# A per-head state in half the columns, y in two PSUM banks, and 14 routing operations on VectorE instead of 17, in a fused attention and mixture-of-experts kernel

## The reference

```python
# 1. linear attention, B=4, H=8, S=768, D=48
cur = einsum('bhd,bhe->bhde', u * k_t, v_t)
y_t = einsum('bhd,bhde->bhe', r_t, state + cur)
state = w * state + einsum('bhd,bhe->bhde', k_t, v_t)
# 2. x = y as (3072, 384); 8 experts, the best one for each token
e_idx = argmax(x @ w_gate);  probs = softmax(x @ w_gate);  eom = sigmoid(x @ w_output_gate)
x2 = probs[e_idx] * eom[e_idx] * (relu(x @ w1[e_idx]) @ w2[e_idx])
# 3. out = (silu(x2 @ w_gate) * (x2 @ w_val)) @ w_out, d_ff = 1536
```

## Time and profile before

| what | us |
|---|---|
| median of the timed executions (3) | 880.84 |
| lowest and highest | 879.64, 881.88 |
| the profiled execution, its own time | 883.9 |
| span of its instructions in the profile | 881.7 |

### The profile page before, as it was taken

One profiled execution on the slowest core, in us unless ns is written; L12 is line 12 of the kernel. 1 busy time (PEld: TensorE's weight loads), 2 busy tenths in 40 slices (PEclk: granted clock), 3 DMA queues, 4 the chain that ended last, 5 costly groups with the idle time before them and its releaser, 6 DMA issues.

```text
span 881.7 us, 16027 instructions
## 1 busy us (share of the span) xinstructions
PE 839.0 (95%) x6056; PEld 763.5 (87%) x6056; DVE 313.0 (35%) x601; ACT 285.9 (32%) x559; POOL 275.5 (31%) x209
## 2 busy tenths in 40 slices
PE   7977998789999999999899999999999999999995
PEld 6876888789999999999788888888888888888885
DVE  6988878632222222221322222322322231222221
ACT  1634444313444444443433212221221222122111
POOL 5857867204555555546242100010010001001001
PEclk9998999779999999999999999999999999999999
DMA  9955564155665467545120000000000000000000
GB/s 186 188 127 137 111 135 101 55 130 149 173 161 144 131 179 177 142 124 163 54 55 0 24 14 1 1 36 0 0 36 0 0 0 36 0 0 36 0 1 37
DMA packets 138889, 67.05 MB, mean 76 GB/s; under 512 B 86232, under 2 KB 136536, under 8 KB 138840
## 3 DMA queue, kind: packets, MB, share of 16 engines
q1 hardware_dynamic: 135768, 56.91, 26.9%
q0 software_dynamic: 3072, 9.45, 2.9%
HBM read 51.76 MB, written 14.59 MB: 75 GB/s over the span
## 4 chain that ended last, share of the span: by engine, by line
PE 86%; DVE 7%; issue 2%; DMA 2%; SPq 1%; another core or an unknown queue 0%; POOL 0%; ACT 0%; POOLq 0%; DVEq 0%
PE bank L1145 25%; PE bank L1147 25%; PE bank L1146 25%; PE bank L1120 2%; PE bank L1099 2%; PE bank L1089 2%; DMA xg<-x_sorted 1%; PE bank L1038 1%; PE bank L1057 1%; PE bank L1043 1%; DVE attn L646 1%; PE bank L1112 1%; PE bank L1154 1%; PE bank L1025 1%; DVE rT L638 1%
## 5 line engine op out<-in xcount | busy, mean ns | idle before, releaser
L531 POOL TENSOR_TENSOR w_lo<-raw,w_hi 128x768 fp32r<-128x768 f32 x64 | 117.9, 1842 | 118.0 <-ACT w_hi L897 118.0
L865 DVE TENSOR_TENSOR act<-silu,bank 128x512 f32<-128x512 f32 x72 | 49.5, 688 | 287.4 <-PE bank L1147 276.7
L584 POOL DMA_INDIRECT out_dram<-o_out,sorted_token x24 | 23.5, 980 | 380.1 <-ACT o_out L1004 374.6
L1146 PE MATMUL bank<-bT,f_hi_late 128*128 (+1 forms) x288 | 112.8, 392 | 0.0
L1147 PE MATMUL bank<-bT,f_lo_late 128*128 (+1 forms) x288 | 112.8, 392 | 0.0
L1145 PE MATMUL bank<-bT,f_hi_late 128*128 (+1 forms) x288 | 112.1, 389 | 0.0
L996 ACT ACTIVATE silu<-bank 128x512 f32<-128x512 f32 x72 | 43.1, 598 | 175.6 <-PE bank L1147 175.6
L998 ACT CAST act_hi<-act 128x512 fp32r<-128x512 f32 x72 | 44.7, 621 | 157.4 <-DVE act L865 157.4
L830 DVE SCALAR_TENSOR_TENSOR h_lo<-bank,h_hi 128x416 fp32r<-128x416 f32 x64 | 37.9, 592 | 149.8 <-ACT h_hi L955 149.8
L955 ACT ACTIVATE h_hi<-bank 128x416 fp32r<-128x416 f32 x64 | 33.2, 518 | 128.2 <-PE bank L1147 128.2
L1145 PE MATMUL bank<-h_hi,w_hi 128*128 128x416 f32 x192 | 69.2, 360 | 0.0
(11 more groups left out here) (168 smaller groups left out, 1642.4 us busy)
## 6 DMA issues: line engine op xcount, KB each, us to landing
raw<-in_moe_w_dram SPq DMA_DIRECT2D x128, 192.0 KB, 3.5
x_sorted<-zeros SPq DMA_DIRECT2D x8, 625.6 KB
xg<-x_sorted SPq DMA_DIRECT2D x8, 625.6 KB
k_in<-in_k_dram SPq DMA_DIRECT2D x24, 192.0 KB
r_in<-in_r_dram SPq DMA_DIRECT2D x24, 192.0 KB
v_in<-in_v_dram SPq DMA_DIRECT2D x24, 192.0 KB
raw<-in_moe_w_gate_dram SPq DMA_DIRECT2D x12, 192.0 KB, 2.6
raw<-in_moe_w_val_dram SPq DMA_DIRECT2D x12, 192.0 KB, 2.8
```

What stands on the lines that cost most here:

```text
L531: pool.tensor_tensor(w_lo[:, f, :], raw[:, f % RAW, 0:WC], w_hi[:, f, :].bitcast(F32), ALU.subtract).then_inc(w_split, 1)
L584: pool.indirect_dma_start(out[:, :], bass.IndirectOffsetOnAxis(sorted_token[:, m * BT + t:m * BT + t + 1].bitcast(U32), 0), o_out[:, t, :] ...
L865: dve.tensor_tensor(act[:, par, :], silu[:, par, :], bank[1][:], ALU.mult).then_inc(act_made, 1)
L1146: pe.matmul(ps, a_hi, b_lo_, start=False, stop=False)
```

## The change

The state of a pair becomes 128 rows by 48 columns, head 2q in the upper rows and head 2q+1 in the lower ones, without the zero blocks. L1099's four matmuls over all rows become eight over half the rows each. Each half writes its own PSUM bank, so y lies in two banks (`y_banks`), even heads in one and odd heads in the other; the router's transposes and logits share the bank that y leaves. In the routing, the arg max is found from `shifted` (is it zero?) in one operation for two, the slot is converted in the reduction that makes it, and the 1 and the 1e-9 of the shares are folded into two-operand instructions: 6, 3 and 5 operations for a group, 14 in place of 17. With two set-up copies `rank_p` and `keep_p`, and with `soft_sum_p` and `ruk_sum`, the small tables lie in PSUM. `choose` moves ahead of the row block in step s+2, `give_shares` goes to step s+4, and the scaling and storing of rows follow. The last two groups are handled behind step 23, and 4 warming matmuls stand where 8 did.

```diff
-state = here("state", [P, B, PAIRS, PW], F32)
+state = here("state", [P, B, PAIRS, D], F32)
...
+def by_parity(t):
+    return t.rearrange("p (q e d) -> p e q d", q=PAIRS, e=2)
+
...
-    return bank[5][:, DM:DM + E * n]
+    return bank[5][:, 2 * P:2 * P + E * n]
+
+
+rank_p = bank[5][:, 448:448 + E]
+keep_p = bank[5][:, 448 + E:448 + E + E * B]
+soft_sum_p = bank[5][:, 448 + E + E * B:448 + E + E * B + B]
+
+ruk_sum = bank[2][:, 0:H]
...
-CHOOSE_AFTER, RANK_AFTER = 2, 3
+CHOOSE_AFTER, RANK_AFTER, SHARE_AFTER = 2, 3, 4
...
-    for b in range(n):
-        step = min(first + n + RANK_AFTER + b // (1 if first < 2 * B else 2), STEPS - 1)
-        if first + n + RANK_AFTER == STEPS - 1:
-            step = STEPS - 1
-        SCALE_IN.setdefault(step, []).append(first + b)
-        STORE_AFTER.setdefault(min(step + 1, STEPS - 1), []).append(first + b)
+    for i in range(first, first + n):
+        step = i + n + SHARE_AFTER
+        SCALE_IN.setdefault(min(step, STEPS), []).append(i)
+        STORE_AFTER.setdefault(min(step + 1, STEPS - 1), []).append(i)
...
-WARM_RANKS, WARM_ROWS, WARM_FIRST = 8, 30, 4
+WARM_RANKS, WARM_ROWS, WARM_FIRST = 4, 30, 4
...
-        dve.tensor_reduce(ruk_sum[:], heads(ruk[:, i % 2, :]), AX.X, ALU.add).then_inc(bonus_sum, 1)
+        dve.wait_ge(masked, 2 * i + 1)
+        dve.tensor_reduce(ruk_sum, heads(ruk[:, i % 2, :]), AX.X, ALU.add).then_inc(bonus_sum, 1)
...
-                          ruk_sum[:].unsqueeze(2).to_broadcast([P, H, D]), ALU.mult).then_inc(bonus_done, 1)
+                          ruk_sum.unsqueeze(2).to_broadcast([P, H, D]), ALU.mult).then_inc(bonus_done, 1)
...
-            delta = bank[5][:, 0:DM].rearrange("p (q n) -> p q n", q=PAIRS)
+            delta = bank[5][:, 0:PAIRS * D].rearrange("p (q n) -> p q n", q=PAIRS)
...
-        dve.tensor_tensor(x_rows(i)[:, 0:DM], bank[4][:, 0:DM], cv[:], ALU.add).then_inc(x_made, 1)
+        dve.tensor_tensor(by_parity(x_rows(i)[:, 0:DM]), y_banks[:, :, 0:PAIRS * D].rearrange("p e (q d) -> p e q d", q=PAIRS),
+                          by_parity(cv[:]), ALU.add).then_inc(x_made, 1)
...
+        done(dve.tensor_copy(rank_p, rank_w[:]))
...
-
-    def choose(g):
+        done(dve.tensor_copy(keep_p, flat(keep_by[B][:])))
+        settle()
+
+    def choose(g, rank, keep):
...
                           ALU.subtract).then_inc(shares_asked, 1)
-        done(dve.tensor_tensor(is_best[:, 0:n, :], gate_l, best[:, 0:n].unsqueeze(2).to_broadcast([P, n, E]),
-                               ALU.is_equal))
-        settle()
-        done(dve.tensor_tensor(ranked[:, 0:n, :], is_best[:, 0:n, :],
-                               rank_w[:].unsqueeze(1).to_broadcast([P, n, E]), ALU.mult))
+        dve.wait_ge(shares_asked, g + 1)
+        done(dve.scalar_tensor_tensor(ranked[:, 0:n, :], shifted[:, 0:n, :], 0.0,
+                                      rank.unsqueeze(1).to_broadcast([P, n, E]), ALU.is_equal, ALU.mult))
         settle()
...
         done(dve.tensor_tensor(chosen_by[n][:], best_rank[:, 0:n].unsqueeze(1).to_broadcast([P, E, n]),
-                               rank_w[:].unsqueeze(2).to_broadcast([P, E, n]), ALU.is_equal))
+                               rank.unsqueeze(2).to_broadcast([P, E, n]), ALU.is_equal))
         settle()
-        dve.tensor_tensor_scan(flat(run_by[n][:]), flat(keep_by[n][:]), flat(chosen_by[n][:]), 0.0,
+        dve.tensor_tensor_scan(flat(run_by[n][:]), keep, flat(chosen_by[n][:]), 0.0,
                                ALU.mult, ALU.add).then_inc(chosen_made, 1)
...
-        done(dve.tensor_reduce(slot_f[:, first:first + n], terms_by[n][:].rearrange("p e b -> p b e"),
-                               AX.X, ALU.add))
-        settle()
-        dve.tensor_copy(slot_i[:, first:first + n], slot_f[:, first:first + n]).then_inc(slots_made, 1)
-
-    def give_shares(g):
+        with nc.allow_low_precision(reason="whole numbers, one other than zero for each token"):
+            dve.tensor_reduce(slot_i[:, first:first + n], terms_by[n][:].rearrange("p e b -> p b e"),
+                              AX.X, ALU.add).then_inc(slots_made, 1)
+
+    def give_shares(g, sums):
...
-        done(dve.tensor_tensor(open_terms[:, 0:n, :], open_exp[:, 0:n, :],
-                               chosen_by[n][:].rearrange("p e b -> p b e"), ALU.mult))
-        done(dve.tensor_reduce(soft_sum[:, 0:n], soft[:, 0:n, :], AX.X, ALU.add))
+        done(dve.tensor_reduce(sums, soft[:, 0:n, :], AX.X, ALU.add))
+        done(dve.scalar_tensor_tensor(open_terms[:, 0:n, :], open_exp[:, 0:n, :], 1.0,
+                                      chosen_by[n][:].rearrange("p e b -> p b e"), ALU.add, ALU.mult))
...
-        done(dve.tensor_scalar(soft_sum1[:, 0:n], soft_sum[:, 0:n], 1e-9, None, ALU.add))
...
-        done(dve.scalar_tensor_tensor(share_den[:, 0:n], open_sel[:, 0:n], 1.0, soft_sum1[:, 0:n],
-                                      ALU.add, ALU.mult))
+        done(dve.scalar_tensor_tensor(share_den[:, 0:n], sums, 1e-9, open_sel[:, 0:n], ALU.add, ALU.mult))
...
-        for g, (first, n) in enumerate(GROUPS):
-            if i == first + n - 1 + RANK_AFTER:
-                give_shares(g)
-                place(g)
-        if i == STEPS - 1:
-            choose(len(GROUPS) - 2)
-        attention_rows(i)
...
-                choose(g)
-    give_shares(len(GROUPS) - 2)
-    place(len(GROUPS) - 2)
-    choose(len(GROUPS) - 1)
-    give_shares(len(GROUPS) - 1)
-    place(len(GROUPS) - 1)
+                choose(g, rank_p, keep_p)
+            if i == first + n - 1 + RANK_AFTER:
+                place(g)
+            if i == first + n - 1 + SHARE_AFTER:
+                give_shares(g, soft_sum_p)
+        attention_rows(i)
+    for g in range(len(GROUPS) - 2, len(GROUPS)):
+        n = GROUPS[g][1]
+        choose(g, rank_w[:], flat(keep_by[n][:]))
+        give_shares(g, soft_sum[:, 0:n])
+        place(g)
...
+    def scale_group(g):
+        first, n = GROUPS[g]
+        for i in range(first, first + n):
+            scale_rows(i)
+
+    late = SCALE_IN[STEPS]
+    scale_rows(late[0])
...
+    scale_rows(late[1])
...
+    scale_rows(late[2])
...
+    scale_rows(late[3])
...
-    first, n = GROUPS[-2]
-    for i in range(first, first + n):
-        scale_rows(i)
+    scale_group(len(GROUPS) - 2)
...
-    first, n = GROUPS[-1]
-    for i in range(first, first + n):
-        scale_rows(i)
+    scale_group(len(GROUPS) - 1)
...
+        wait(pe, logit_copied, i)
...
-            mm = pe.transpose(bank[6][:, c * P:(c + 1) * P], x_rows(i)[:, c * P:(c + 1) * P], ident[:])
+            mm = pe.transpose(bank[4][:, c * P:(c + 1) * P], x_rows(i)[:, c * P:(c + 1) * P], ident[:])
...
+        wait(pe, bonus_done, i)
...
             for q in range(PAIRS):
-                pe.matmul(bank[4][:, q * PW:(q + 1) * PW], rT[:, q * P:(q + 1) * P], state[:, b, q, :],
-                          start=(q == 0), stop=False, skip_group_check=True)
+                for half in range(2):
+                    pe.matmul(y_banks[:, half, q * D:(q + 1) * D], head_rows(rT, half, q), state[rows_of(half), b, q, :],
+                              start=(q == 0), stop=False, skip_group_check=True)
         if i < STEPS - 1:
...
-                mm = pe.matmul(bank[5][at:at + D, h * D:(h + 1) * D], k_pad[:, par, h, 0:D],
+                q = h // 2
+                mm = pe.matmul(bank[5][at:at + D, q * D:(q + 1) * D], k_pad[:, par, h, 0:D],
...
+            q = h // 2
...
-                mm = pe.matmul(bank[4][rows_of(half), h * D:(h + 1) * D], attn[:, h % 2, h // 2, rows_of(half)],
+                mm = pe.matmul(y_banks[rows_of(half), h % 2, q * D:(q + 1) * D], attn[:, h % 2, q, rows_of(half)],
...
-                               start=(c == 0 and h == 0), stop=(h == H - 1),
+                               start=(c == 0 and q == 0), stop=(q == PAIRS - 1),
...
     logits_turn(STEPS - 1)
+    logits_mm(STEPS - 1)
     ranks(len(GROUPS) - 2)
-    logits_mm(STEPS - 1)
-
     stay_warm(WARM_RANKS, bank[0])
```

More of the change, by code:

```diff
@@ L57, in build @@
     PAIRS = H // 2
-    PW = 2 * D
     E = w_gate.shape[1]
@@ L170, in build @@
         slot_i = here("slot_i", [P, NT], I32)
-        slot_f = here("slot_f", [P, NT], F32)
         best = here("best", [P, B], F32)
         best_rank = here("best_rank", [P, B], F32)
-        is_best = here("is_best", [P, B, E], F32)
         ranked = here("ranked", [P, B, E], F32)
@@ L181, in build @@
         soft_sum = here("soft_sum", [P, B], F32)
-        soft_sum1 = here("soft_sum1", [P, B], F32)
         open_terms = here("open_terms", [P, B, E], F32)
@@ L242, in build @@
         assert cursor[0] <= pair_at
-        bank = [ctx.enter_context(nc.psum_tensor(f"bank{i}", [P, 512], F32)) for i in range(8)]
+        bank = [ctx.enter_context(nc.psum_tensor(f"bank{i}", [P, 512], F32)) for i in range(6)]
+        y_banks = ctx.enter_context(nc.psum_tensor("y_banks", [P, 2, 512], F32))
+        bank += [y_banks[:, 0, :], y_banks[:, 1, :]]
         def sem(name):
```

7 lines of the change are left out of this document (3 added, 4 removed).

## The result

| what | before | after |
|---|---|---|
| median of the timed executions | 880.92 (4) | 873.3 (4) |
| lowest and highest | 879.64, 881.88 | 872.49, 875.25 |
| the profiled execution, its own time | 883.9 | 873.29 |
| its span | 881.7 | 871.1 |

The ratio is 0.993, with a 95% interval of 0.9913 to 0.9947: faster, as predicted, but by 7.6 us and not by 20. The forecast was 860.5 and its range ended at 869. All times are us.

What follows compares the result with a forecast made beforehand. Bound: the chain in the first 183 us, where VectorE's routing waits for GpSimd and TensorE for x_out. Gains 16.9 + 1.0 + 0.4 = 18.3, plus 1.8 at the end: 20.1 off 880.84, forecast 860.5 us, range 853 to 869.

Steps and rivals of the forecast that it cites:

- Part 1, the three tables that moved: Steps 4 to 19: cv, ranked and chosen get a PSUM input, L748 goes; 14.3 us of waiting go.
- Part 1, the stalls that stay: Steps 4 to 19: shifted and open_terms keep 5.3 us of waiting, hidden by the order except 1.6 in all.
- Steps 20 to 22: Steps without state update: 15.4 us instead of 15.8, a gain of 0.4.
- The first rival: Remaining shifted and open_terms stalls delay x_out and TensorE: 1.3 us at each of eight places, about 869; chance 0.17.
- The clock: Granted clock on the steps up to 23: full speed expected as a sign, no time set aside for dips.
- Part 2: The state matmuls L1099 as eight half matmuls on TensorE: +0.2 us a step.
- rival 2: Half the rows halve L1099's time to 0.53 us, step 5.04: about 852; chance 0.08.
- Steps 0 to 3: First four steps: two table copies cost 0.4 us against four cv stalls of 0.4; a gain of 1.0.
- The end: From step 23's scores to the read of the sorted rows: 1.8 us shorter besides the nameless wait.
- the nameless wait: After step 23, x_out waits 3.55 us for something the profile can't name; taken as absent from the timed runs.

Runs made afterwards that it cites:

- number 12: A kernel of its own without the computation: 1, 3 or 6 GpSimd products beside small VectorE additions, second input in SBUF or PSUM; PSUM pair 0.22 us.
- number 7: Changed kernel with ruk_sum, rank_w, keep and soft_sum read from SBUF again, the rest of the change kept: 892.3 us, ratio 1.0079 to the kernel before.
- number 4: Kernel before with only the row sums ruk_sum in PSUM (and the scores' wait for bonus_done): 881.0 us, ratio 0.9953.
- number 2: Changed kernel with best, a copy of the one-hot that open_terms reads, and seen also in PSUM: 862.85 us, ratio 0.974 to the kernel before.
- number 9: Changed kernel with dummy matmuls ahead of L1112's wait for x_out, 4 in steps s+3 and 3 in steps s+5: 868.88 us, ratio 0.9873 to the kernel before.
- number 3: Changed kernel with best and shifted placed ahead of rT in step s+2, both inputs in SBUF: 867.74 us, ratio 0.9797 to the kernel before.
- number 8: Kernel of number 2 with the state in its old form (96 columns with zero blocks, y in one bank): 863.32 us, ratio 0.9756 to the kernel before.
- number 11: Kernel of number 8 with 7 dummy matmuls on TensorE in step 1 ahead of the wait for x_out: 855.53 us, ratio 0.972 to the kernel before.
- number 5: The changed kernel again, unchanged, on another chip: 877.06 us, ratio 0.9917 to the kernel before.
- 1: Changed kernel with the row maximum best written to PSUM, so that shifted has one SBUF input: 864.26 us, ratio 0.9749 to the kernel before.
- 6: Changed kernel with 8 dummy matmuls on TensorE ahead of L1112's wait for x_out in steps s+3 and s+5: 880.89 us, ratio 0.9968 to the kernel before.
- 10: Changed kernel, tables untouched, with GpSimd waiting for x_out before its products in three steps of a group: 864.42 us, ratio 0.9838 to the kernel before.

## Why the prediction missed

**Part 1, the three tables that moved: right.** `cv` 554 ns, `ranked` and `chosen` 187, whatever GpSimd does; number 12 shows the same alone. Of the 14.3 us that I counted, 11.2 were theirs and 3.1 those of L748; number 7 puts the tables at 15.2, with executions from 888.9 to 898.8. The reason I gave, that all their waiting lies on the path, is not right: `cv`'s is mostly free (number 4), and what does lie on the path comes with half clock behind it (number 7).

**Part 1, the stalls that stay: the step that failed.** It reads: "with the mean stall of `shifted` at 6.2, done by 6.8 ... So `choose` fits, unless its stall is far above the mean", and "I leave 0.4 us a group for stalls above the mean, 1.6 in all". The mean came from the old place, behind `x_out`, where `shifted` took 0.19 to 1.04 us. In the new place both are released by the same event, the end of the state's matmuls, so the old mean says nothing about it: in nine of ten groups of the two traces of the changed kernel it takes 0.58 to 2.26. In the trace after it measured 1.27 of waiting for 0.54, in the mean of four groups. `open_terms` went from 0.8 to 0.9, and `seen`, two SBUF inputs on 8 numbers, was left out of my list because it happened to take 162 ns before. In place of 1.6 us, S(4) to S(20) lost 9.2 to the three: it takes 99.9, and 90.7 with them in PSUM (number 2). Steps 20 to 22 lost another 3.5 to the `shifted` of the fifth group (18.7 and 15.2), for which I had left nothing. The first rival named this mechanism at 0.17. Its price, 1.3 for each of eight places, about 869, was also short: TensorE waited 0.95 to 1.36 in four places only, and the clock behind them cost more than the waits.

**The clock: left out.** I wrote that a clock at full speed up to step 23 would be seen, and no term stood for anything else, although show its dips before. In the trace after, three idle times of TensorE of 1.25 to 1.36 us were each followed by 6.8 us at 1.2 GHz; number 9 puts these at 8 us in all, so this is the larger half of the price. Idle time is not enough by itself: 2.02 us of it in the trace before (136.5 to 138.5) and 1.94 in number 3 were followed by no half clock for 12 us and more. What decides between them stays open.

**Part 2: right, a size off.** I took +0.2 us a step for L1112; it is 1.02 for 0.86 and the plain step 5.49 for 5.38, +0.11, which gave 1.3 us back in 16 steps. That the zero blocks save nothing on TensorE held (number 8), and rival 2's half time did not show.

**Steps 0 to 3: wrong by 1.7.** I forecast 1.0 saved, and 0.7 was lost. S(2) came at 23.95 for 23.25, with 3.4 us at half clock (20.4 to 23.8) behind TensorE's idle time in step 1, 6.8 in other executions; with dummy matmuls there S(4) is 31.86 (number 11, in the old form of the state).

**The end: 19.2 for 19.1, partly by luck.** The same kernel takes 22.7 there in number 5, most of it at half clock (147.2 to 171.1). I took it that the timed executions don't have the nameless wait of 3.55, and that doesn't hold in general: the trace after doesn't have it, but those of numbers 1, 2, 3, 6, 7 and 8 have one of 2.3 to 3.8 ahead of `terms`, and the profiled execution of number 2 takes its median all the same (863.0 and 862.85). Those of numbers 9, 10 and 11, on the third chip, have none. What ends it stays open; in the trace of number 2 no transfer of the instruction queue stands between 144 and 150 us, where the wait lies.

**What stays open.** In the kernel an operation can wait for two products (2.26), in number 12 the first one never did. In the traces of numbers 1, 3, 5, 6, 7, 9 and the changed kernel `shifted`, `open_terms` and `seen` take 1.7 us and more 19 times. Each of these starts between 0.44 ahead of `k_pad` and 0.24 behind its start, with a scatter (L558) that ends directly ahead of `k_pad`; from 0.25 behind it on it is one product (0.58 to 0.82). One wait without a scatter ahead, 0.22 behind `k_pad`, took only 0.84. This suggests that the scatter has a part in it; it wasn't tried apart. Nor were the tables in PSUM with the routing in its old place, where TensorE and VectorE would have touched one bank at once.

The Trainium skill, "SBUF — State Buffer", section "Who interferes with whom", gave the right rule for the two-input instructions here. With both inputs in SBUF the small ones took up to 2.45 us; with one in PSUM they kept their plain time in every trace. For one SBUF input the page rules contention out only outside VectorE's two-port modes, which it says `tensor_scalar` can enter. My prediction left that condition out and said that the rows agree, though L748, with one SBUF input, is among them. In the trace before it waits:

```profile
81.44 1.81 POOL L531 TENSOR_TENSOR w_lo<-raw,w_hi 128x768 fp32r<-128x768 f32 x1
81.80 1.48 DVE L748 TENSOR_SCALAR soft_sum<-soft_sum 128x4 f32<-128x4 f32 x1
```

The rule says whom it hits; how long, and where on the path, only the timeline told.

## What to carry to other kernels

List every VectorE instruction with two SBUF inputs that will stand between TensorE's last matmul and what TensorE waits for, also the tiny ones and those that were short in the trace, and give one input a place in PSUM. When an instruction is moved, don't price its wait by its old mean: ask which event releases it in the new place, and whether the same event starts the other engine. And look at the granted clock behind each idle time of TensorE: three of some 1.3 us cost about 8 us more here, while others as long cost nothing more. A few dummy matmuls in the gap held the clock; where nothing was late they cost their own time.
